# Order of GpSimd and VectorE work in the first group, and first tiles centred by row sums, in a fused linear-attention and expert kernel

## What is computed

```
state, y per head:  y[t] = r[t] @ (state + (u*k[t]) v[t]^T);  state = w*state + k[t] v[t]^T
x   = y as rows of 384;  xn = (x - mean(x)) / sqrt(var(x) + 1e-6) * g
x2  = x + relu(xn @ w_ch1) @ w_ch2                         (384 -> 1536 -> 384)
out = p[e] * (relu(x2 @ w1[e]) @ w2[e]),  e: one of 8 experts per token, with a sticky gate
```

## Time and profile before

| | |
|---|---|
| median of 3 runs | 396.76 us (396.62 to 397.79) |
| profiled execution: time, span | 395.23 us, 393.4 us |
| busy share of TensorE, VectorE, ScalarE, GpSimd | 96%, 58%, 41%, 33% |
| chain that ended last, by engine | TensorE 90%, GpSimd 3%, VectorE 2% |

### The profile page before, as it was taken

The page is one execution under the profiler, slowest core; times in us unless marked ns, Lnnn a source line. Parts: engine busy times, 40 slices in busy tenths (PEclk is TensorE's granted clock), DMA queues, the critical chain, the costliest instruction groups (busy, mean ns, idle before and its releaser), DMA issues.

```text
span 393.4 us, 9032 instructions
## 1 busy us (share of the span) xinstructions
PE 379.2 (96%) x3193; PEld 345.4 (88%) x3193; DVE 227.3 (58%) x464; ACT 161.3 (41%) x299; POOL 128.0 (33%) x113
## 2 busy tenths in 40 slices
PE   8997999999999999999999999999999999999992
PEld 6887999999999999999999855789999999999982
DVE  7877944524623452464477759698656665547440
ACT  5555312413231241323243255187625852555520
POOL 2887861830650262000001203502332233223231
PEclk9999999999999999999999999999999999999998
DMA  7996312400331240500008396699892478111011
GB/s 216 334 330 154 103 43 87 130 20 20 109 105 40 80 133 20 182 2 22 22 0 315 90 310 190 186 374 315 290 349 93 142 237 310 42 33 45 24 44 42
DMA packets 32634, 54.91 MB, mean 140 GB/s; under 512 B 3261, under 2 KB 20323, under 8 KB 32592
## 3 DMA queue, kind: packets, MB, share of 16 engines
q1 hardware_dynamic: 30288, 48.07, 37.8%
q0 software_dynamic: 2304, 6.30, 5.2%
HBM read 49.64 MB, written 5.51 MB: 140 GB/s over the span
## 4 chain that ended last, share of the span: by engine, by line
PE 90%; POOL 3%; DVE 2%; issue 1%; ACT 1%; DMA 1%; SPq 0%; POOLq 0%; DVEq 0%; ACTq 0%
PE bank L1020 18%; PE bank L920 6%; PE bank L922 6%; PE bank L921 6%; PE bank L1351 5%; PE bank L1323 5%; PE bank L1359 5%; PE bank L1355 5%; PE bank L1330 5%; PE bank L1327 5%; PE bank L1340 3%; PE bank L935 3%; PE bank L1252 3%; PE bank L1229 3%; PE bank L964 2%; PE bank L954 2%
## 5 line engine op out<-in xcount | busy, mean ns | idle before, releaser
L1020 PE MATMUL bank<-xnT_hi,parts 128*128 128x256 f32 x432 | 66.6, 289 | 1.4 <-ACT xnT_hi L703 0.6
L1020 PEld LDWEIGHTS bank<-xnT_hi,parts 128*128 128x128 f32 x432 | 56.5, 191 | 3.4 <-ACT xnT_hi L703 0.9
L648 POOL DMA_INDIRECT out_y<-late x14 | 20.4, 1459 | 94.0 <-DVE late L1878 94.0
L1534 DVE SCALAR_TENSOR_TENSOR parts<-bank,parts 128x512 fp32r<-128x512 f32 x36 | 24.8, 690 | 43.6 <-ACT parts L710 43.6
L920 PE MATMUL bank<-parts 128*128 128x384 f32 x144 | 49.1, 341 | 0.0
L922 PE MATMUL bank<-parts 128*128 128x384 f32 x144 | 48.2, 335 | 0.0
L921 PE MATMUL bank<-parts 128*128 128x384 f32 x144 | 48.1, 334 | 0.0
L796 ACT ACTIVATE parts<-stage (+1 forms) x32 | 46.2, 1486 | 2.7 <-DMA stage<-in_w 2.4
L1847 DVE TENSOR_TENSOR parts<-stage,parts x24 | 41.1, 1754 | 5.2 <-ACT parts L796 4.5
L710 ACT ACTIVATE parts<-bank 128x512 fp32r<-128x512 f32 x36 | 21.5, 597 | 55.2 <-PE bank L1020 54.7
L1020 PE MATMUL bank<-xnT_lo,parts 128*128 128x256 f32 x216 | 37.3, 282 | 0.0
(11 more groups left out here) (250 smaller groups left out, 734.0 us busy)
## 6 DMA issues: line engine op xcount, KB each, us to landing
stage<-in_w SPq DMA_DIRECT2D x36, 768.0 KB, 6.9
stage<-in_w_ch SPq DMA_DIRECT2D x6, 768.0 KB, 8.5
arena<-in_k_t SPq DMA_DIRECT2D x12, 224.0 KB, 3.7
arena<-in_r_t SPq DMA_DIRECT2D x12, 224.0 KB, 3.0
arena<-in_v_rows SPq DMA_DIRECT2D x12, 192.0 KB, 4.2
arena<-in_k_rows SPq DMA_DIRECT2D x12, 192.0 KB, 3.5
x_rows<-stage SPq DMA_DIRECT2D x12, 192.0 KB, 1.9
arena<-in_r_rows SPq DMA_DIRECT2D x10, 192.0 KB, 3.3
```

What stands on the lines that cost most here:

```text
L648: pool.indirect_dma_start(out, bass.IndirectOffsetOnAxis(give[:, s:s + 1], 0), yo[s % 2], None, bounds_check=T - 1, oob_is_err=False).then ...
L1020: mm = pe.matmul(acc, w[:, k, at], x[:, k, :], start=start and k == 0, stop=stop and k == KD - 1, skip_group_check=first and q == 0)
L1534: dve.scalar_tensor_tensor(hT_lo[:, at, :].rearrange("p a t -> p (a t)"), bk[6 + q % 2][:], 0.0, hT_hi[:, at, :].rearrange("p a t -> p (a ...
```

## The change

- Tiles 0 and 1 (`first_rows`): the addition also gives the row sum (`accum_out`); a one-column multiply makes the mean, and ScalarE centres by it (`first_centred`). `bn_stats` and `bn_aggr` of these tiles (`first_stats`, `means(0)`), ScalarE's `deviation(0)` and VectorE's `scales(0)` move into group 0.
- GpSimd: pieces 0 and 1 both in halves, directly one behind the other; end products of chunk 2, then piece 2 (VectorE's before), then decays and rows.
- VectorE: `first_group` takes the place of the `first` branches: `scales(0)` stands behind `coefs(2)`, ahead of `hidden` step 3 and the masks of chunk 3; pieces 3 and 5 come behind `rows_of(2)` and `new_state(3)`.
- ScalarE: the second half of piece 0 is rounded before tile 1 is turned, piece 4 before the state's decay of chunk 3.
- Waits of TensorE and SP follow the new counts of `lo_p` (6 in all) and `lo_v` (2).

```diff
-LO_V = 2, 3, 5
+LO_V = 3, 5
+LO_P = 6
...
             def piece(i):
                 if i >= 4:
-                    if i == 4:
-                        sp.wait_ge(lo_p, 2)
-                    else:
-                        sp.wait_ge(lo_p, 3)
+                    sp.wait_ge(lo_p, 2 if i == 4 else 4)
...
-            def first_piece(half):
-                pool.wait_ge(hi_done, half + 1)
+            def half_piece(i, half):
+                pool.wait_ge(hi_done, half + 1 if i == 0 else i + 2)
...
             ends(1)
-            first_piece(0)
-            first_piece(1)
+            for i in range(2):
+                for half in range(2):
+                    half_piece(i, half)
+            ends(2)
+            rest_of_piece(2)
+            pool.wait_ge(rdec_ready, 3)
             pool.wait_ge(kdec_ready, 3)
-            rest_of_piece(1)
-            ends(2)
+            decays(3)
             pool.wait_ge(s_u, 16)
             rows(2)
+            ends(3)
             diagonal(2)
-            decays(3)
+            rest_of_piece(4)
             rows(3)
-            ends(3)
             diagonal(3)
-            pool.wait_ge(lo_v, 2)
-            rest_of_piece(4)
...
+            def first_centred(u):
+                act.wait_ge(s_mean0, u + 1)
+                act.activation(xn[u], tile_of(u), ACT.Identity, bias=mean0[:, u:u + 1], scale=-1.0).then_inc(xn_ready, 1)
...
                 hidden(g, range(2, 3))
                 if first:
+                    act.wait_ge(s_eps, 1)
+                    act.wait_ge(mean_ready, B)
+                    deviation(0)
                     round_piece(3)
...
-                decay(g * 2 + 3, 1)
                 if first:
                     round_piece(4)
+                decay(g * 2 + 3, 1)
...
             for u in range(2):
-                centre_tile(0, u)
+                first_centred(u)
+            round_first(1)
             act.wait_ge(s_ng, 1)
             turned_tile(0, 1)
-            round_first(1)
             round_piece(1)
-            act.wait_ge(s_eps, 1)
-            deviation(0)
...
                         if first and half == 0:
-                            if q < 3:
+                            if q < 5:
                                 pe.wait_ge(lo_p, q + 1)
-                            elif q == 4:
-                                pe.wait_ge(lo_v, LO_V.index(2) + 1)
...
+            def first_rows(c, bank):
+                dve.wait_ge(y_mm, c + 1)
+                dve.wait_ge(cv_ready, c + 1)
+                dve.scalar_tensor_tensor(tile_of(c), bank[:, 0:DM], 1.0, cv[c], ALU.mult, ALU.add,
+                                         accum_out=sum0[:, c:c + 1]).then_inc(x_ready, 1)
+                dve.wait_ge(x_ready, c + 1)
+                dve.tensor_scalar(mean0[:, c:c + 1], sum0[:, c:c + 1], 1.0 / DM, None, ALU.mult).then_inc(s_mean0, 1)
+
+            def first_stats():
+                for u in range(B):
+                    dve.bn_stats(stats[:, u, :], tile_of(u)).then_inc(stats_ready, 1)
...
+            def first_group():
+                hidden(0, range(0, 1))
+                new_state(0, 0, bk[3])
+                hidden(0, range(1, 2))
+                masked(2, bk[0:2], scT[0])
+                new_state(1, 1, bk[2])
+                first_stats()
+                means(0)
+                hidden(0, range(2, 3))
+                new_state(2, 0, bk[3])
+                coefs(2, 0)
+                scales(0)
+                hidden(0, range(3, 4))
+                masked(3, bk[0:2], scT[0])
+                rows_of(2, 0, bk[4])
+                rest_of_piece(3)
+                hidden(0, range(4, 5))
+                new_state(3, 1, bk[3])
+                rest_of_piece(5)
+                coefs(3, 1)
+                hidden(0, range(5, NHP))
+                rows_of(3, 1, bk[4])
+                means(1)
+                rows_done(0)
...
-            rows_of(0, 0, bk[4])
-            mean(0, 0)
-            rows_of(1, 1, bk[5])
-            mean(0, 1)
+            first_rows(0, bk[4])
+            first_rows(1, bk[5])
             first_turned()
             turned(0, range(1, 2))
             third_decays()
-            group(0)
+            first_group()
```

More of the change, by code:

```diff
@@ L154, in build_program @@
         mv = sb("mv", [P, B, 2])
+        sum0, mean0 = sb("sum0", [P, B]), sb("mean0", [P, B])
         vare, root, rstd0, sq, rstd = (sb(n, [P, NT]) for n in ("vare", "root", "rstd0", "sq", "rstd"))
@@ L276, in build_program @@
         s_pair, s_k1, s_hi0, s_wc = sem("s_pair"), sem("s_k1"), sem("s_hi0"), sem("s_wc")
+        s_mean0 = sem("s_mean0")
         s_v = [sem(f"s_v{u}") for u in range(2)]
@@ L472, in _ @@
             sp.wait_ge(lo_v, len(LO_V))
-            sp.wait_ge(lo_p, 4)
+            sp.wait_ge(lo_p, LO_P)
             sp.wait_ge(rt_v, RT_CHOSEN)
@@ L568, in rest_of_piece @@
                                    ALU.subtract).then_inc(lo_p, 1)
-            def first_piece(half):
-                pool.wait_ge(hi_done, half + 1)
+            def half_piece(i, half):
+                pool.wait_ge(hi_done, half + 1 if i == 0 else i + 2)
                 at = slice(half * GT, (half + 1) * GT)
-                pool.tensor_tensor(piece_at(0, 1)[:, :, at], piece_stage(0)[:, :, at],
-                                   piece_at(0, 0)[:, :, at].bitcast(F32), ALU.subtract).then_inc(lo_p, 1)
+                pool.tensor_tensor(piece_at(i, 1)[:, :, at], piece_stage(i)[:, :, at],
+                                   piece_at(i, 0)[:, :, at].bitcast(F32), ALU.subtract).then_inc(lo_p, 1)
             pool.memset(eps[:], LN_EPS).then_inc(s_eps, 1)
@@ L1066, in rows_out @@
                     if isinstance(g, int) and g == 0 and u == 0 and f % 4 == 0:
-                        pe.wait_ge(*((lo_p, 4) if f == 4 else (lo_v, LO_V.index(KD + f // 4) + 1)))
+                        pe.wait_ge(*((lo_p, LO_P) if f == 4 else (lo_v, LO_V.index(KD + f // 4) + 1)))
                     if between and f % 4 == 3:
@@ L1600, in rest_e @@
                                   ALU.subtract).then_inc(e_lo[j // EP], 1)
+            def first_group():
[22 more added lines that the diff above has]
+                rows_done(0)
             def group(g, ends=True):
-                first = isinstance(g, int) and g == 0
                 hidden(g, range(0, 1))
[L1605 to L1608, removed]
+                coefs(g * 2 + 2, 0)
                 hidden(g, range(1, 2))
                 masked(g * 2 + 2, bk[0:2], scT[0])
-                if first:
-                    new_state(1, 1, bk[2])
-                    coefs(g * 2 + 2, 0)
                 hidden(g, range(2, 3))
@@ L1616, in group @@
                     new_state(g * 2 + 2, 0, bk[3])
-                if first:
-                    rest_of_piece(2)
                 rows_of(g * 2 + 2, 0, bk[4])
@@ L1622, in group @@
                 masked(g * 2 + 3, bk[0:2], scT[0])
-                if first:
-                    rest_of_piece(3)
                 hidden(g, range(4, 5))
@@ L1630, in group, with rows_done @@
                 hidden(g, range(5, NHP))
-                if first:
-                    rest_of_piece(5)
-                    scales(0)
+                rows_done(g)
+            def rows_done(g):
                 if isinstance(g, int) and g == NG - 2:
```

## The result

The changed kernel takes 401.77 us (median; 401.17 to 402.29) beside 397.17 for the kernel before: ratio 1.0115, interval 1.0092 to 1.0138, so it is slower by 1.2%. A second series gave 401.31 beside 395.12, ratio 1.0142 (1.0111 to 1.0174). In the first series the profiled execution of the changed kernel took 401.64 us with a span of 399.8, 6.4 us more than the profiled execution before.

A forecast was written before the change was run, and what follows sets the result against it. TensorE, busy 96% of the span, was taken as the bound. Profiled 395.23 + 3.95 (late state products) + 2.0 (clock) = 401.2, standing 1.5 us under the median, so 402.7 against 396.76; range 396.1 to 404.2.

The forecast's parts named there:

- Opening: Tiles 0 and 1: ScalarE centres tile 0 0.3 to 0.5 us sooner, yet group 0 still begins at 17.4; counted zero.
- GpSimd's sum: GpSimd's work from 15.25 added up: 17.2 us, so decays 3 done at 30.4 and row products 2 at 32.4.
- TensorE up to chunk 3: Piece stalls go; scores of chunk 3 begin at 30.45 instead of 33.26, TensorE ready for state products at 34.3.
- The small steps: `scales(0)` on VectorE: dependent steps each meet a GpSimd instruction, taking 0.2, 0.8, 3.4 and 0.9 us.
- The term of +3.95 us: State products of chunk 3 on TensorE begin at 41.05 instead of 37.08, as `x_ready` 3 comes late.
- What is not held: VectorE's reciprocal in `scales(0)` was claimed not to be held by GpSimd.
- Diagonal 2: GpSimd's 0.83 us instruction (L557) was taken to hold VectorE fully, to 34.25; no row showed whether it does.
- The not-slower rival: Diagonal 2 does not hold, or piece 4 is rounded after 34.4: net -0.45 us, 396.3; chance 0.17.
- the clean chain: VectorE from row products 2 to `x_ready` 3 without holds: 3.9 us, `x_ready` at 36.35, state products at 36.4.
- The clock: TensorE's clock falls to 1.2 GHz in the 6.8 us wait; +2.0 us, the middle of nothing and +3.9.
- it stands 1.5 us under the median: The profiled execution before, 395.23, against the median 396.76; the step taking the forecast from 401.2 to 402.7.
- The sum against the profiled execution: Profiled execution before plus both terms: 395.23 + 3.95 + 2.0 = 401.2 us.

The follow-up runs named there:

- opening_alone: The kernel before with only the row-sum opening and the later statistics of tiles 0 and 1; 396.54 us beside 396.11, ratio 1.0015.
- scales_last: The changed kernel with the five small steps of `scales(0)` back at the end of group 0; 394.42 us beside 396.00 for the kernel before.
- piece4_later: The changed kernel with GpSimd's piece 4 moved behind row products 3; 397.39 us beside 396.00 for the kernel before, ratio 1.0046.
- second pair: The changed kernel again, beside it with 40 warming matmuls ahead of the wait of chunk 3's state products: 401.31 and 399.51 us.
- before_warm: The kernel before with 14 warming matmuls in its 2.0 us wait ahead of chunk 3's scores; 394.57 us beside 396.09, ratio 0.9962.

## Why the prediction was right, and where it was not

The forecast was 402.7 in a range of 396.1 to 404.2; measured, 401.77.

- **Opening.** Forecast: nothing to be had. Measured none: the 0.09 us at the start of group 0 stand ahead of the changed instructions already, and `opening_alone` shows no difference. Tile 0 was centred 0.7 us sooner (forecast 0.3 to 0.5) without any use. The accumulator costs a read of 0.08 us (taken as 0.1). The one-column multiply took 0.15 us beside diagonal 1 and was not held.
- **GpSimd's sum.** Forecast: decays 3 done at 30.4, row products 2 at 32.4. Measured 30.19 and 32.25.
- **TensorE up to chunk 3.** Forecast: scores at 30.45, ready for the state products at 34.3. Measured 30.24 and 34.24.
- **The small steps.** Forecast 0.2, 0.8, 3.4 and 0.9 us; measured 0.30, 0.75, 3.35, 0.91. `x_ready` was due at 41.05 and came at 40.74. The term of +3.95 us measured +3.81. `scales_last` and `piece4_later` confirm the cause: the steps away from there remove the wait but for 1.1 us, a shorter instruction in the way shortens it.
- **What is not held.** The prediction says that the reciprocal is not held, for which no row of before stands; here it took 0.16 us inside end products 3, so it is right.
- **Diagonal 2,** for which no row of before spoke, does hold VectorE: the second step ended with it, within 0.01 us. The not-slower rival thus fell at the point that it named. Its other terms were good: the clean chain gave 35.50 in `scales_last` where 36.4 less the 0.95 for the steps was due.
- **The clock.** Forecast +2.0, the middle of two bounds 3.9 us apart; measured 2.5 in the first profile, 2.0 by the second pair. That the middle came this near is luck: no row told how soon the clock comes back. And my picture of when was wrong: from the end of the trace before I read that the clock falls 5.0 us into idleness, and expected 0.5 from about 39 to 44. It was low from about 36.2, 2 us in, to 46.4, and from 38.9 to 45.7 in another execution.
- **The step that was mis-sized** is the last one, from the profiled execution to the median: "it stands 1.5 us under the median". I added the whole 5.95 us to the median of before as if that offset were a constant. `before_warm` shows that it is largely a clock that falls around the 2.0 us stall, which the change removes. The sum against the profiled execution (401.2) was 0.4 us short of its measured 401.64; the one against the median 0.9 us too long. The two errors, 0.5 us too little for the clock and 1.5 too much for the offset, partly cancel.

## What to carry to other kernels

Before moving small dependent steps on VectorE, list what GpSimd runs beside them: here four steps of 0.16 us took 5.3 us, each waiting for the GpSimd instruction beside it, and the longest of these (3.43 us) made most of it. Put such steps into a wait that is already there, or behind the instruction that others wait for. Ask what the clock does in TensorE's waits, even in one as short as the 2.0 us here, and compare medians with medians: one profile may come from an execution in which the clock did not fall.

## What the hardware showed that I had not expected

- The granted clock fell 2 us into one wait and 4.6 us into the same wait of the same kernel in another execution. It stayed at 1.00 through 3.5 us in the profile of `piece4_later`. With its wait of 2.0 us, 47 of 74 executions of the kernel before have a mean clock under 0.994; with the wait filled, none of 12 has. Where it fell within those executions no profile shows.
- After the products had begun again at 40.89, the clock came back only at about 46.4, 5.5 us later; in the second profile it took 4.7 us (41.01 to 45.7).
- A `tensor_scalar` of 128x2 elements was held (0.94 us in the earlier trace rows, 3.35 here), one of 128x1 was not: it took 0.15 us inside diagonal 1. Nor was a reciprocal of 128x2, 0.16 us inside end products 3. Why they differ was not tried.
- GpSimd is held in the same way: L536 took 2.40 us instead of 1.02 beside VectorE's piece 2.
